# Other costs, one other size and one other dependency in the planner that orders a kernel for attention and two feed-forward layers

## The reference, cut to what matters

```
q_d, k_d, v_d = means over groups of 4 tokens          # 144 groups
out_up    = repeat(softmax(q_d k_d^T / 8) v_d, 4)      # attention between groups
out_local = softmax over |i - j| < 4 of q k^T / 8, v   # band of 7 keys
x = (out_up + out_local), as 2304 tokens x 512
h = x @ w_in (512 x 2048);   g = s * relu(h)**2 + b;   x2  = g @ w_out (2048 x 512)
h = x2 @ w_in2;              g = h - tanh(h);          out = g @ w_out2
```

## Time and profile before

| | us |
|---|---|
| median of 3 runs | 921.44 (921.01 to 922.37) |
| the profiled execution | 921.01 |
| its span, first to last instruction | 919.2 |

### The profile page before, as it was taken

One profiled execution on the slowest core, in us unless ns is written; L12 is line 12 of the kernel. 1 busy time (PEld: TensorE's weight loads), 2 busy tenths in 40 slices (PEclk: granted clock), 3 DMA queues, 4 the chain that ended last, 5 costly groups with the idle time before them and its releaser, 6 DMA issues.

```text
span 919.2 us, 15706 instructions
## 1 busy us (share of the span) xinstructions
PE 900.0 (98%) x6129; PEld 847.8 (92%) x6129; DVE 500.4 (54%) x627; ACT 423.4 (46%) x1058; POOL 298.7 (32%) x288
## 2 busy tenths in 40 slices
PE   8998999999999999999999999999999999999997
PEld 7788999999999899999999999999999999999996
DVE  5649679999999989871003632423323323322322
ACT  3897675556654664437456722323223223222221
POOL 6567573998399942634222000000000000000000
PEclk9999999999999999999999999999999999999999
DMA  8961653433344322003025400200200100100101
GB/s 227 263 230 32 168 136 68 110 91 97 96 112 96 95 70 47 24 6 125 1 73 183 164 1 1 70 1 1 70 1 20 51 1 0 35 1 1 35 1 35
DMA packets 48238, 65.17 MB, mean 71 GB/s; under 512 B 18150, under 2 KB 29988, under 8 KB 48164
## 3 DMA queue, kind: packets, MB, share of 16 engines
q1 hardware_dynamic: 46916, 62.59, 24.5%
q10 hardware_dynamic: 1248, 1.57, 0.6%
HBM read 54.71 MB, written 9.44 MB: 70 GB/s over the span
## 4 chain that ended last, share of the span: by engine, by line
PE 79%; DVE 7%; POOL 4%; ACT 4%; issue 2%; SPq 2%; DMA 1%; DVEq 0%; ACTq 0%; POOLq 0%
PE acc L1884 21%; PE hid L1866 21%; PE acc L1847 16%; PE hid L1819 15%; DVE prod L1248 2%; POOL own L987 1%; DVE prod L1256 1%; POOL gl L1010 1%; POOL xl L1001 1%; DVE prod L1261 1%; PE pa L1777 1%; DMA wa_raw<-in_moe_w_in_dram 1%; ACT pc L1451 1%; SPq L847 1%; PE pa L1761 1%
## 5 line engine op out<-in xcount | busy, mean ns | idle before, releaser
L1010 POOL TENSOR_TENSOR gl<-relu,gh 128x288 fp32r<-128x288 f32 x128 | 128.0, 1002 | 180.3 <-PE acc L1847 114.9
L1847 PE MATMUL acc<-gh,wbh 128*128 128x288 f32 (+1 forms) x512 | 154.1, 301 | 0.1
L1819 PE MATMUL hid<-xh,wah 128*128 128x288 f32 x512 | 153.7, 302 | 0.2 <-ACT relu L1536 0.2
L1315 DVE TENSOR_TENSOR gdif<-hid,tanh 128x384 f32<-128x384 f32 x96 | 53.5, 557 | 182.1 <-ACT tanh L1577 181.9
L1847 PE MATMUL acc<-gl,wbh 128*128 128x288 f32 (+1 forms) x512 | 151.5, 296 | 0.0
L1847 PE MATMUL acc<-gh,wbl 128*128 128x288 f32 (+1 forms) x512 | 151.2, 295 | 0.0
L1819 PE MATMUL hid<-xh,wal 128*128 128x288 f32 x512 | 150.5, 295 | 0.0
L1819 PE MATMUL hid<-xl,wah 128*128 128x288 f32 x484 | 142.2, 295 | 0.0
L1577 ACT ACTIVATE tanh<-hid 128x384 f32<-128x384 f32 x96 | 47.1, 491 | 186.6 <-PE hid L1866 186.6
L1866 PE MATMUL hid<-x2h,wah 128*128 128x384 f32 x384 | 129.1, 336 | 0.3 <-DVE gdif L1315 0.3
L1866 PE MATMUL hid<-x2h,wal 128*128 128x384 f32 x384 | 129.1, 336 | 0.0
(11 more groups left out here) (152 smaller groups left out, 1563.4 us busy)
## 6 DMA issues: line engine op xcount, KB each, us to landing
wa_raw<-in_moe_w_in_dram SPq DMA_DIRECT2D x8, 1024.0 KB, 7.7
wb_raw<-in_moe_w_out_dram SPq DMA_DIRECT2D x8, 1024.0 KB, 5.6
kl<-in_k_dram SPq DMA_DIRECT2D x23, 240.0 KB
vl<-in_v_dram SPq DMA_DIRECT2D x23, 240.0 KB
x2T<-ystage SPq DMA_DIRECT2D x8, 576.0 KB, 3.2
x2raw<-x2T SPq DMA_DIRECT2D x6, 768.0 KB, 4.5
own<-in_q_dram SPq DMA_DIRECT2D x11, 384.0 KB
own<-in_k_dram SPq DMA_DIRECT2D x9, 384.0 KB
```

The costliest lines, as they stand in the source:

```text
L1010: g.tensor_tensor(out=gl[:, turn % LRING1, 0:NS], in0=relu[:, f % 2, :], in1=gh[:, turn % GRING1, 0:NS].bitcast(F32), op=ALU.subtract).the ...
L1315: ve.tensor_tensor(gdif[:, f % 2, :], hid[:, f % 2, 0:N2], tanh[:, f % 2, :], ALU.subtract).then_inc(s_dif, 1)
L1819: one = pe.matmul(dst, w[:, d, cols], x[:, j % XRING, d, :], start=i == 0, stop=i == 3 * KT - 1)
L1847: one = pe.matmul(acc[:, d, n], w[:, f, cols], g[:, turn % ring, n], start=(f == 0 and p == 0), stop=(f == FT - 1 and p == 2))
```

## The change

It gives four groups of TensorE steps other costs in the plan: `dense_scores` 1.25 for 0.75, `dense_values` 0.85 for 0.75, `late_scores` 1.0 for 0.75, `late_values` 0.9 for 0.8. It gives the first six group loads of batch 0 a planned size of 140 for 200 KB. And in the plan the first `key_products` of the band on VectorE depends on the last `late_values` and no longer on the last `late_add`. No instruction's own work and no wait written in the kernel's engine programs changes.

```diff
-        o.add("PE", 0.75, (0, 0, 3 + 1), ("dense_scores", a), [("dense_keys", a), ("dense_queries", a)]
+        o.add("PE", 1.25, (0, 0, 3 + 1), ("dense_scores", a), [("dense_keys", a), ("dense_queries", a)]
...
-        o.add("PE", 0.75, (0, 0, 3 + 3), ("dense_values", a), [("dense_place", a), ("load_dense_values",)]
+        o.add("PE", 0.85, (0, 0, 3 + 3), ("dense_values", a), [("dense_place", a), ("load_dense_values",)]
...
-        o.add("PE", 0.75, (0, 0, 21), ("late_scores", a), [("late_keys", a), ("late_queries", a)]
+        o.add("PE", 1.0, (0, 0, 21), ("late_scores", a), [("late_keys", a), ("late_queries", a)]
...
-        o.add("PE", 0.8, (0, 0, 23), ("late_values", a), [("late_place", a, 1), ("load_late_values",), ("place_up", 0, NPAIR + a)],
+        o.add("PE", 0.9, (0, 0, 23), ("late_values", a), [("late_place", a, 1), ("load_late_values",), ("place_up", 0, NPAIR + a)],
...
-                  kbytes=(240 if b else 200) if n < 6 else 180)
+                  kbytes=(240 if b else 140) if n < 6 else 180)
...
-                  [("load_queries", s), ("load_keys", s)] + ([("late_add", NPAIR - 1)] if s == SB else []),
+                  [("load_queries", s), ("load_keys", s)] + ([("late_values", NPAIR - 1)] if s == SB else []),
```

## The result

The changed kernel is slower: median 928.59 us (926.2 to 932.74, 7 runs) beside 921.66 us (921.01 to 923.22, 7 runs) for the kernel before, a ratio of 1.0078 with a 95% interval of 1.0055 to 1.0101, that is 5.1 to 9.3 us. Its profiled execution took 928.84 us.

A forecast was written before the change was run, and what follows sets the result against it. TensorE was taken as the bound (busy 900.0 of 919.2 us), after attention work up to hidden1(0,0). Terms 1.6 + 0 + 3.3 + 0 = 4.9 us on 921.0 gave 925.9, median 926.2; range 922.4 to 929.5.

The forecast's parts named there:

- the hold at the landing: ScalarE at the front: both weight roundings wait for the load landing at 29.68, putting 1.2 us of work behind it.
- the late order: Last late steps: late_values(3) comes after output1(0,12) and the product ahead of late_add(3); TensorE idles 3.3 us.
- part 2: From 43 to 95 us: TensorE's order stays until late_scores(3); cost 0, bounds -1.5 and +1.5 us.
- the fall of the clock: Rival: half clock after a 2.3 us idle piece of TensorE, 3.2 us more, 929.4; chance 0.05.
- Part 1, the front: Ahead of hidden1(0,0): roundings go before dense_place(1) and dense_exp(2); 1.6 us later, at 45.1, bounds 0.6 and 2.6.
- What I had called hidden: Up to 25 us: group_sums ahead of dense_keys(1), 141 dummy transposes for 155; some 0.5 us, hidden by the landing.
- Part 3, the last late steps: Around output1(0,12) to hidden1(1,0): late_values(3) and late_add(3) lose their cover; 3.3 us, bounds 0.3 and 4.5.
- My lower bound for it: Last late steps: 0.3 us if late_values(3) stays ahead of output1(0,12), with late_add(3) moving by 2.48 us.
- Part 4, the band: VectorE's band starts 5.1 us later, TensorE 4.9; later waits stay about the same: 0, bounds -3.3 and +1.5 us.
- front only: Rival: late_values(3) keeps its cover, so only the front costs; 923.3, or 922.4 with the front's lower bound; chance 0.18.
- nothing: Rival: the order of instructions changes only where there is slack; 921.4 us; chance 0.06.
- faster: Rival: softmax of batch 1 done sooner, waits at about 204 and 317 us go; 920.0 or 919; chance 0.07.

The follow-up runs named there:

- the two runs with the changed front and no fall: Changed kernel with the cost of late_scores back at 0.75 (1.0077); changed kernel's plan with late_add(3) moved back ahead of key_products(2,0) (1.0063).
- the pair that differs in the front alone: Changed kernel with late_scores back at 0.75 (1.0077), beside kernel before with only the first key_products' dependency changed (1.0043); 3.1 us between them.
- the front's swap in the old plan: Kernel before, whole plan kept, only w1_high(0,0) and w1_high(1,0) moved ahead of dense_place(1) in ScalarE's list: 1.0032, 3.0 us above before.
- the run with both repairs: Changed kernel with 14 more dummy transposes ahead of dense_turn(2), and w1_high(0,0) and w1_high(1,0) moved behind dense_exp(2) on ScalarE: 1.0056.
- the run with the raised size: Changed kernel with the planned size of the first weight load raised from 620 to 980 KB: 1.0061, 5.6 us above the kernel before.
- the run with dummies: Changed kernel with 20 dummy transposes right before scores(1,1), keeping TensorE at work in the wait on the last late_add: 1.0052.
- the run with the add first: Changed kernel's plan kept, only late_add(3) moved back ahead of key_products(2,0) in VectorE's list: 1.0063.

## Why the prediction was right, and where its sizes were off

Forecast 926.2 with 922.4 to 929.5, measured 928.59; the size, on the profiled execution, 4.9 of 7.8 us. The two mechanisms, the hold at the landing and the late order, are as forecast. That the time lies inside the range is partly luck: part 2 fell outside its own bounds, and the fall of the clock that I had given 0.05 came.

- *Part 1, the front.* Order and hold as written: both roundings ahead of the two copies, landing unmoved. 1.6 forecast, 2.3 measured at `hidden1(0,0)`, within the bounds. One trace is less sure than that: the old order of the front has 43.47, 43.55, 44.28 and 44.75 in four kernels, the new one 45.77, 45.82, 45.90 and 45.91, so on average 1.8. What I had called hidden (the turned order on VectorE) cost 2 us up to 27.6 and not 0.5, because the wait of 1.66 us it caused was followed by half clock (in the two runs with the changed front and no fall the copies ended at 25.7 and 26.1). It was covered by the landing all the same. That a delay here reaches the end is shown by the pair that differs in the front alone (3.1 us for 1.5 at `hidden1(0,0)` in its traces) and by the front's swap in the old plan (3.0 us), and supported by the run with both repairs (2.0 us for 1.5, intervals overlapping).
- *Part 2, the middle.* This is the term that was mis-sized: 0 with bounds of 1.5 either way, measured 2.1. I had put it at nothing for the order alone and had not followed the loads. The order up to `late_scores(3)` was as I had it. TensorE's waits from 46 to 112 us sum to 4.6 for 3.0 us, mainly `late_values` on the `lkT` copy (1.5 for 0.8) and a new one of 1.1 us for the group sums `ks`. The last load they need was issued at 97.84 and had landed at 104.66 before; now it was issued at 101.10 and landed at 109.0. This wait depends on the landing: with the same late order it was 0.5 us in the run with both repairs and none in the run with the raised size, whose load landed at 108.2. The other 0.5 us I have not traced.
- *Part 3, the last late steps.* The order of TensorE and VectorE came out as worked out, step for step. `hidden1(1,0)` was due 6.35 us after `output1(0,12)` and came 7.05 after; 3.3 us of loss forecast, 4.0 measured, and 1.2 more inside the two slow groups behind it. The excess is the product (3.03 us for the row's 2.48) and `scores(1,1)` at half clock (1.30 for 0.98): where the trace has neither, in the run with the raised size, it came after 6.2 us. The price of the product ahead of the add is, however, not what I made of it. With the rest of the plan kept it is 0.6 us in the order of before and some 1.4 in the late order, although 3.5 us go at the place: VectorE's band sets the pace when TensorE doesn't. My lower bound for it was right in size and wrong in reason, since I had left out the buffer.
- *Part 4, the band.* Forecast 0, measured 0.6 given back. The two waits on the band that the prediction places at about 204 and 317 us lie at 207 and 306 us; in the changed kernel waits of 0.9 and 0.8 us stand for them. But this was not known from the rows: the same edits taken one by one drew later waits of up to 3.3 us that the full change doesn't have. A bound of 1.5 us above was too narrow for a planner that reorders everything behind an edit.
- *The clock.* I gave it 0.05 as a rival of its own. It came true besides the forecast, twice. At the front it was covered. In the late place it costs 1.5 us, where I had 3.2: 9.40 us for 7.87 with the same idle piece and the same product. The run with dummies agrees (1.9, less 0.3 for the product). Over all runs it may be more: the mean granted clock is 0.9926 over the changed kernel's runs and 0.9974 over 23 later runs of the kernel before, and 0.0048 of 925 us is 4.4 us, an estimate of the most that half clock can take from TensorE, covered places included. The Trainium skill's page TensorE: Matmul & The Clock Gate, Part 1: The HAM clock gate, says that idle time sends the engine back to half rate. The trace agrees in that each of its two falls has an idle piece right ahead of it, of 1.66 and of 2.58 us; but such a piece was not followed by a fall each time.

The rival "front only" fell with the rows of part 3, "nothing" and "faster" with the result. It stays open how much the late order alone costs: the one run of it, 6.2 us, contains later orders and two falls of the clock of its own.

## What to carry to other kernels

A cost in a planner is not a model to be made more exact: it selects an order, and each change of it shuffles everything behind. To price one swap, keep the plan and move that one step; to price a plan, time it. Where an engine waits for a landing with ready work behind, try the ready work first (1.3 us here by the medians). And look at what a wait does to TensorE's clock before calling it small.

## What the runs showed of the hardware

The length of the idle piece alone did not tell whether the clock falls. The clearest pair is the late place of two runs, with 2.04 us of idle and the same steps around it: 1.00 after it in the run with the raised size, 0.63 in the run with both repairs. It fell to half after pieces of 1.66 and 2.58 us in the changed kernel, while pieces of 1.6 and 1.7 us in the kernel before left it at 1.00. And the wait of 1.5 us for `lkT` left it at 1.00 in the changed kernel and was followed by 0.60 in the run with dummies and by 0.57 in the run with the add first, where nothing ahead of it on any engine had been changed. Eight matmuls of 288 columns took 1.92 us for 1.05 at half clock. The changed kernel's runs lie 6.5 us apart and those of the kernel before 2.2 us; every run's mean granted clock is on record, and it differs with the time: 0.989 in the changed kernel's slowest run (932.74 us), 0.994 and 0.996 in its two fastest (926.2 and 926.56 us). An estimate: from 0.989 to 0.996 half clock can take 0.007 of 927 us, 6.5 us, and these two lie 6.2 us apart. So how long an execution runs at half clock changes from run to run of one kernel; where in it the falls lie is known of the profiled one alone.
